# A two-stage mixture-of-experts pipeline on one core: the second stage's rows are added into the output by the scatter itself

## The reference

```python
x = attention(q, k, v, lam)                # 1536 rows of 512
# stage 1: each row goes through one of 8 experts
out[mask] = gate_w[mask, None] * (np.maximum(x[mask] @ w1[e], 0.0) @ w2[e])
# stage 2: each row goes through two of 8 other experts, chosen by noisy logits
for e in range(8):
    for k in range(2):
        mask = top2[:, k] == e
        h = np.maximum(x[mask] @ w1[e], 0.0)
        out[mask] += top2_w[mask, k, None] * (h @ w2[e])
```

## Time and profile before

| what | before |
| --- | --- |
| median of 3 runs | 727.5 us (727.25 to 727.71) |
| the profiled execution, its own time | 730.47 us |
| its span on the core | 728.7 us |
| PE busy | 661.3 us (91%) |
| DVE busy | 351.1 us (48%) |
| ACT busy | 295.7 us (41%) |
| POOL busy | 195.6 us (27%) |
| chain that ended last | PE 85%, DMA 5%, DVE 4%, issue 3%, ACT 2% |

### The profile page before, as it was taken

How to read it: one execution, slowest core, us unless ns; L and a number is a source line. 1 busy time by engine, 2 the same in 40 slices (tenths; PEclk the granted TensorE clock), 3 DMA queues, 4 the chain that set the end, 5 groups by cost and what they waited for, 6 DMA issues and landing times.

```text
span 728.7 us, 13666 instructions
## 1 busy us (share of the span) xinstructions
PE 661.3 (91%) x3733; PEld 533.3 (73%) x3734; DVE 351.1 (48%) x623; ACT 295.7 (41%) x443; POOL 195.6 (27%) x291
## 2 busy tenths in 40 slices
PE   2999379999999999872899999999999999999994
PEld 1888258888888888551588888888888888888883
DVE  3887674564556556117632626235244444522211
ACT  2444634464556446062522626235234444422220
POOL 2000021222122222100322434444343534433332
PEclk9999689999999999985999999999999999999998
DMA  6976777755575561452541545516336372212110
GB/s 203 373 277 222 249 258 297 244 171 205 199 240 179 195 218 44 151 183 82 173 162 58 183 148 172 185 58 227 106 90 233 95 247 68 69 58 58 44 58 19
DMA packets 40003, 118.44 MB, mean 163 GB/s; under 512 B 9533, under 2 KB 10557, under 8 KB 38413
## 3 DMA queue, kind: packets, MB, share of 16 engines
q1 hardware_dynamic: 27222, 89.51, 36.1%
q0 software_dynamic: 10608, 28.08, 11.8%
q10 hardware_dynamic: 2154, 0.60, 0.4%
HBM read 103.40 MB, written 18.43 MB: 167 GB/s over the span
## 4 chain that ended last, share of the span: by engine, by line
PE 85%; DMA 5%; DVE 4%; issue 3%; ACT 2%; POOL 0%; SPq 0%; POOLq 0%; DVEq 0%; ACTq 0%
PE bank L750 11%; PE bank L771 11%; PE bank L752 11%; PE bank L770 11%; PE bank L751 11%; PE bank L772 11%; PE bank L759 5%; PE bank L741 3%; PE bank L644 2%; PE bank L637 2%; PE bank L624 1%; DMA xrow<-x_d,picked_ids 1%; PE bank L670 1%; DVE at_row L1017 1%; DMA x_all<-x_d 1%
## 5 line engine op out<-in xcount | busy, mean ns | idle before, releaser
L750 PE MATMUL bank<-W,xTh 128*128 (+1 forms) x360 | 150.9, 419 | 5.2 <-DVE xTl L1063 2.8
L770 PE MATMUL bank<-W,hTh 128*128 x360 | 142.8, 397 | 1.4 <-DVE yrow L1079 0.8
L771 PE MATMUL bank<-W,hTh 128*128 x360 | 143.5, 399 | 0.0
L752 PE MATMUL bank<-W,xTl 128*128 (+1 forms) x360 | 143.1, 398 | 0.0
L751 PE MATMUL bank<-W,xTh 128*128 (+1 forms) x360 | 142.4, 396 | 0.0
L772 PE MATMUL bank<-W,hTl 128*128 x360 | 142.3, 395 | 0.0
L520 ACT ACTIVATE hrow<-bank 128x512 f32<-128x512 f32 x90 | 53.6, 596 | 156.9 <-PE bank L752 156.9
L524 ACT CAST hTh<-bank 128x512 fp32r<-128x512 f32 x90 | 52.8, 587 | 152.4 <-PE bank L759 152.4
L1069 DVE TENSOR_TENSOR hTl<-bank,hTh 128x512 fp32r<-128x512 f32 x90 | 62.1, 689 | 96.8 <-ACT hTh L524 96.7
L1063 DVE TENSOR_TENSOR xTl<-bank,xTh 128x512 fp32r<-128x512 f32 x47 | 32.5, 692 | 128.0 <-ACT xTh L516 128.0
L770 PEld LDWEIGHTS bank<-W,hTh 128*128 128x128 f32 x360 | 67.9, 189 | 19.0 <-issue 2.4
(11 more groups left out here) (162 smaller groups left out, 638.8 us busy)
## 6 DMA issues: line engine op xcount, KB each, us to landing
raw<-moe_w_dram SPq DMA_DIRECT2D x64, 512.0 KB, 6.1
x_all<-moe_w_dram SPq DMA_DIRECT2D x64, 512.0 KB, 6.1
qkv<-att_in_dram SPq DMA_DIRECT2D x12, 1024.0 KB, 6.8
x_d<-x_all SPq DMA_DIRECT2D x12, 256.0 KB, 7.5
out_dram<-zeros SPq DMA_DIRECT2D x1, 3072.0 KB, 13.4
x_all<-x_d SPq DMA_DIRECT2D x12, 256.0 KB, 5.9
xrow<-x_d,picked_ids POOLq DMA_INDIRECT x45, 4.1
gate_row<-gates_d,picked_gate POOLq DMA_INDIRECT x29
```

Of the source, the lines that this page charges most:

```text
L750: pe.matmul(h_ps[half][:, :], xTh[:, k, :], hi, start=(k == 0), stop=False)
L752: last = pe.matmul(h_ps[half][:, :], xTl[:, k, :], hi, start=False, stop=(k == KD - 1))
L770: pe.matmul(y_ps[:, :], hTh[:, k, :], hi, start=(k == 0), stop=False)
L771: pe.matmul(y_ps[:, :], hTh[:, k, :], lo, start=False, stop=False)
```

## The change

`acc`, its memset, its semaphores and `fetch_out` are gone. The scatter of a finished tile carries `compute_op=ALU.add`: the DMA adds `yrow` to the rows that stand in the output. VectorE's operation has no second tensor: y times gate. It waits for the gates (`gate_in_row`) and for `sum_free`, which Pool raises once the tile before has landed, since `yrow` is read by that DMA. The target's indices are copied just ahead of the wait for the finished tile. Pads are no longer left out: each of a tile's 128 places has a spare row of its own (`spare_row`, rows 1536 to 1663), so the output in DRAM has 128 more rows, zeroed with the others, and the host drops them.

```diff
+            nc.gpsimd.iota(spare_row[:, :], pattern=[[0, 1]], base=TT * P + 1, channel_multiplier=1,
+                           allow_small_or_imprecise_dtypes=True)
...
-                         zeros[:, :].unsqueeze(1).to_broadcast([P, TT, D])).then_inc(zeroed, 16)
+                         zeros[:, :].unsqueeze(1).to_broadcast([P, TT + 1, D])).then_inc(zeroed, 16)
...
-            def fetch_out(g):
+            def add_out(g):
 
                 pick_target(1, g)
-                nc.gpsimd.indirect_dma_start(
-                    out=acc[:, :], out_offset=None, in_=out,
-                    in_offset=bass.IndirectOffsetOnAxis(ap=picked_target[:, 0:1], axis=0),
-                    bounds_check=TT * P - 1, oob_is_err=False).then_inc(acc_in, 16)
-
-            def store_out(g):
-
                 pool.wait_ge(y_kept[1], g + 2)
                 pool.sem_inc(pool_passed, 1)
                 nc.gpsimd.indirect_dma_start(
                     out=out, out_offset=bass.IndirectOffsetOnAxis(ap=picked_target[:, 0:1], axis=0),
                     in_=yrow[:, :], in_offset=None,
-                    bounds_check=TT * P - 1, oob_is_err=False).then_inc(y_stored[1], 16)
+                    bounds_check=(TT + 1) * P - 1, oob_is_err=True, compute_op=ALU.add).then_inc(y_stored[1], 16)
 
-            def out_stored(g):
+            def out_added(g):
                 pool.wait_ge(y_stored[1], g * 16 + 16)
-                pool.sem_inc(pool_passed, 1)
+                pool.sem_inc(sum_free, 1)
 
             def pass_on(g):
-                store_out(g)
+                add_out(g)
                 fetch_gate(g + 1)
-                out_stored(g)
-                fetch_out(g + 1)
+                out_added(g)
...
-                step(nc.vector.tensor_scalar(is_pad[:, 0:GMAX[s] + 1], source[s][:, :], 0.0, float(8 * TT * P),
+                past_all = float(8 * TT * P) if s == 0 else spare_row[:, 0:1]
+                step(nc.vector.tensor_scalar(is_pad[:, 0:GMAX[s] + 1], source[s][:, :], 0.0, past_all,
...
-                    dve.wait_ge(acc_in, g * 32 + 32)
-                    nc.vector.scalar_tensor_tensor(out=yrow[:, :], in0=y_ps[:, :], scalar=gate_row[:, 0:1], in1=acc[:, :],
-                                                   op0=ALU.mult, op1=ALU.add).then_inc(y_kept[s], 1)
+                    dve.wait_ge(sum_free, g + 1)
+                    dve.wait_ge(gate_in_row, g * 16 + 16)
+                    nc.vector.tensor_scalar(yrow[:, :], y_ps[:, :], gate_row[:, 0:1], None, ALU.mult).then_inc(y_kept[s], 1)
...
-    out = nc.dram_tensor("out_dram", (B * S, H * DH), F32, kind="ExternalOutput").ap()
+    out = nc.dram_tensor("out_dram", (B * S + 128, H * DH), F32, kind="ExternalOutput").ap()
```

More of the change, by code:

```diff
@@ L78, in moe_pipeline @@
         lane = sb("lane", [P, 1])
+        spare_row = sb("spare_row", [P, 1])
         first_of = sb("first_of", [P, 2 * TT], BF16)
@@ L153, in moe_pipeline @@
         xTh, xTl = sb("xTh", [P, KD, P], F32R), sb("xTl", [P, KD, P], F32R)
-        xrow, yrow, acc = sb("xrow", [P, D]), sb("yrow", [P, D]), sb("acc", [P, D])
+        xrow, yrow = sb("xrow", [P, D]), sb("yrow", [P, D])
         at_byte = [W_at]
@@ L194, in moe_pipeline @@
         gate_picked, target_kept, yrow_free = sem("gate_picked"), sem("target_kept"), sem("yrow_free")
-        gates_spread, gates_stored, acc_cleared, acc_in = (sem(n) for n in ("gates_spread", "gates_stored", "acc_cleared", "acc_in"))
+        gates_spread, gates_stored, gate_in_row = (sem(n) for n in ("gates_spread", "gates_stored", "gate_in_row"))
+        sum_free = sem("sum_free")
         x_stored, rows_cleared, x2_stored = sem("x_stored"), sem("rows_cleared"), sem("x2_stored")
@@ L397, in fetch_gate @@
                     out=gate_row[:, :], out_offset=None, in_=gates_d,
-                    in_offset=bass.IndirectOffsetOnAxis(ap=picked_gate[:, 0:1], axis=0)).then_inc(acc_in, 16)
-            def fetch_out(g):
+                    in_offset=bass.IndirectOffsetOnAxis(ap=picked_gate[:, 0:1], axis=0)).then_inc(gate_in_row, 16)
+            def add_out(g):
                 pick_target(1, g)
-                nc.gpsimd.indirect_dma_start(
-                    out=acc[:, :], out_offset=None, in_=out,
-                    in_offset=bass.IndirectOffsetOnAxis(ap=picked_target[:, 0:1], axis=0),
-                    bounds_check=TT * P - 1, oob_is_err=False).then_inc(acc_in, 16)
-            def store_out(g):
                 pool.wait_ge(y_kept[1], g + 2)
@@ L441, in _ @@
             pool.sem_inc(x2_stored, 1)
-            nc.gpsimd.memset(acc[:, :], 0.0).then_inc(acc_cleared, 1)
+            pool.sem_inc(sum_free, 1)
             pool.wait_ge(source_kept, 2)
@@ L452, in _ @@
             fetch_gate(0)
-            fetch_out(0)
             fetch_next(1, 1)
@@ L458, in _ @@
             pass_on(last_tile - 1)
-            store_out(last_tile)
-            out_stored(last_tile)
+            add_out(last_tile)
+            out_added(last_tile)
         @block.scalar
@@ L1229 @@
     r = run_bass_kernel_spmd(nc, [arrays], core_ids=[0])
-    return r.results[0]["out_dram"]
+    return r.results[0]["out_dram"][:B * S]
```

1 line of the change is left out of this document (removed).

## The result

| what | before | after |
| --- | --- | --- |
| median | 727.46 us, 4 runs (727.25 to 727.71) | 732.86 us, 4 runs (730.44 to 734.12) |
| ratio | 1 | 1.007 (1.0043 to 1.0097) |
| profiled execution, its span | 730.47, 728.7 us | 730.44, 728.5 us |

A forecast was written before the change was run, and what follows sets the result against it. TensorE, busy 91% of the span, bounds the kernel, so only the end counts: VectorE's earlier start (-2.15), shorter operation (-0.06) and slower last landing (+1.5) give -0.7 us, 727.5 to 726.8 us. Range 724.0 to 729.4.

The forecast's parts named there:

- the end of the sum: Span's end: last tile's VectorE start 2.15 us earlier, operation 0.06 shorter, last landing 1.5 longer; -0.7 us in all.
- 0.97 behind: Span's end: 0.97 us left between the last scatter's landing, taken as about 2.3 us, and the end.
- The late 3.22 us: Pool's queue at tile 27's scatter: late code, 2.7 us too much, moving to the gates' fetch for tile 28.
- The landing: Last adding scatter: lands in 3.8 us, bounds 2.8 to 5.5, against about 2.3 before; +1.5 us.
- one sign of being wrong: Last adding scatter: the forecast is wrong if the landing is far from 3.8 us.
- the 693 ns of a copy: VectorE's operation on `yrow`: 751 ns becomes about stage 1's PSUM copy time, -0.06 us for the last one.
- my 2.70: Last gates' gather, tile 28: given the 2.70 us of the other gather, landing at 721.65.
- TensorE's 356.8 of 359 us: Stage 2: TensorE busy for 356.85 of 359 us, so it waited only 2.15 us for anyone.
- the absence of any loss in the loop: Stage 2's loop: its 28 tiles give nothing and cost nothing, 0 us.
- the 34.2 us: Stage 2: VectorE's 11 late waits for old output rows, not worth 34 us because TensorE did not wait.
- rival B: Last tiles: slow add, 8.4 us landing, +4.9 us, 732.4; decides from 6.0 us, about 6.7 without late code; chance 0.16.
- no change: Whole kernel: a time within 1.5 us, about 0.2%, of the kernel before; chance 0.42.

The follow-up runs named there:

- e2: Changed kernel with the addition (compute_op) taken off its scatter; ratio to before 1.0051.
- e5: Changed kernel with one Pool drain between stage 2's loop and the last two tiles; ratio to before 0.9983.
- e9: Changed kernel with pads left out and a Pool drain at the end of every turn of stage 2's loop; ratio to before 0.9969.
- e4: Changed kernel, still adding, with pads left out by the bounds check; ratio to before 1.0022.
- e6: Kernel before with one Pool drain between stage 2's loop and the last two tiles; ratio to before 1.0003.
- e10: Kernel before with a Pool drain at the end of every turn of stage 2's loop; ratio to before 1.025.
- e3: Kernel before, unchanged, run again; ratio to before 1.0002.
- e8: Kernel before with one more gather of 128 rows on Pool between the stages; ratio to before 1.0048.
- e11: Changed kernel with a single Pool drain between the two stages; ratio to before 1.0047.
- e16: e9 with the addition taken off its scatter; ratio to before 0.9932.
- e12: Kernel before with a Pool drain in every turn of stage 2 and behind the loop, between the scatter's landing and `fetch_out`; ratio to before 1.035.
- e15: Kernel before with a Pool drain in every turn of stage 2's loop, between `fetch_next` and `pass_on`; ratio to before 1.0019.

## Why the prediction was wrong

**The step that failed is the end of the sum.** I took "0.97 behind" the last landing for a constant. It held Pool's closing drain of 0.64 us, and that became 3.99. No view that I had read shows the drain; it shows under line 53, and as the difference between the last landing and the span's end. e2, e5 and e9 show that it is variable and can be moved: 7.50, 0.29, 0.29. What in the change lengthened it stays open: without the addition it is longer still (e2), and without the pads it is the same 3.99 (e4).

**The late 3.22 us: wrong cause, and so a wrong place.** I read it as code that comes late at a fixed place, and forecast that 2.7 us of it would reappear ahead of the gates' fetch for tile 28. There the queue takes its plain 0.5 us. Instead 1.0 us stands at the last scatter. A drain in front removes the lateness wherever it stood (e5, e6, e10), and in the kernel before a turn in the middle of the loop, at 606 us, has a stretch of 1.34 us too where 0.53 is plain, in code that has run many times. The packet of the queue "instruction" misled me: e3 is late by the same 3.22 us and its trace shows no such packet there. The Trainium skill, Runtime: NRT & Kernel Launch, "Instruction fetch mechanics", speaks against a stall in straight code; on that point it was nearer to the result than my reading. How Pool decides when to pay stays open: e8 and e11 exclude a plain count.

**The landing: right in kind, short in size.** Forecast 3.8, bounds 2.8 to 5.5; the last add with pads took 4.95, with pads left out 3.86. The pads were in the sum, since 3.8 stood for a full tile; the reading was priced too low. I gave it 1.0 us over the plain scatter's 2.8, and a full add takes 4.9 in the median, 2.1 over. So the step was +2.5 for my +1.5, and one sign of being wrong, a landing far from 3.8, had come. The traffic of e2's last scatter, then of the changed kernel's, each in 40 slices of 0.2 us:

```profile
GB/s 0 0 0 0 0 0 0 0 0 0 0 0 0 307 328 451 225 0 0 0 0 0 0 0 0 0 0 0 0 0 0 0 0 0 0 0 0 0 0 0
DMA packets 80, 0.26 MB, mean 33 GB/s; under 512 B 16, under 2 KB 16, under 8 KB 80
```

```profile
GB/s 0 0 0 0 0 0 0 0 0 0 0 0 72 92 113 154 41 0 123 205 184 195 123 10 0 0 0 0 0 0 0 0 0 0 0 0 0 0 0 0
DMA packets 144, 0.26 MB, mean 33 GB/s; under 512 B 16, under 2 KB 16, under 8 KB 144
```

Without 16 small ones, 64 packets in four slices have become 128 in eleven. The Trainium skill, Collectives: The Full Stack, "The bandwidth ceiling", says of the add in a collective that it emits one descriptor for each source, two where a copy has one, and so runs at half the rate. The doubled packets agree; the time does not: 0.8 us became 2.2, nearly three times as much.

**Unforeseen in size.** The adding scatter holds Pool 1.61 us where the plain one takes 1.02, which I had kept equal. VectorE's operation did not get shorter: 751 ns with one tensor as with two, where I took the 693 ns of a copy. The last gates landed in 3.21 us for my 2.70. Together 1.2 us.

**What held.** TensorE's 356.8 of 359 us and the absence of any loss in the loop; the 34.2 us that are worth nothing there; rival B's threshold was not reached, as the last tile is released by the gates at 716.67 and not by the add. The time came out near B's 732.4 by another mechanism. Without the drain's 3.35 us the tail would have been equal to that of before, which lies in "no change".

Measured, -3.6 + 1.0 + 2.5 + 3.35 = +3.3 us of tail. The medians differ by 5.4 (3.1 to 7.1 by the interval), and in the second set of runs by 0.55%, 4.0 us (2.5 to 5.6). The 3.3 lies within both; that the rest is scatter from ahead of stage 2 fits, but is not shown.

## What to carry to other kernels

A span's end is part of the sum: subtract the last landing from it, and ask what stands between. Where GpSimd issues many indirect DMAs, look for stretches that wait for nothing in its queue and at its closing drain, and try a drain of your own in each turn, at a place where no large gather is in flight and the engine idles anyway. Price a change at the end only when this put-off work is out of the way: with it, a saving of 3.6 us (e2) vanished; without it, and with pads left out, taking the addition away was worth 1.5 (e16).

## What the hardware showed that I had not expected

- Work of Pool's DMA queue that is put off: a drain takes 2.76 us after 33 DMAs (e11), 3.33 after 40 (e9), 7.25 after 118 (e5; the gates' gather landed at its start). The closing drain takes 0.21 us when two DMAs stand between it and the drain before (e12), 0.29 with three (e5, e9), 0.39 with five (e6), 0.62 with eight (e15). What is not drained turns up as stretches of up to 3.22 us at an issue, where 0.54 is plain, and in the close: 0.64, 3.99 or 7.50 us, of which the first two came out the same to the nanosecond in two sets of runs.
- Pool's drain also waits for its DMAs in flight: in e9 all but the first end 0.17 us behind a landing, in e10 and e15 0.21. With a gather of 128 rows just issued it takes 3.8 us in the median and up to 7.8 while weights are loaded (e10).
- An adding scatter of 128 rows of 2 KB: 1.61 us of issue for 1.02, twice the packets, 2.2 us of traffic for 0.8, and 4.9 us to land in the median for 2.8.
